# Two slot tiles of the first three batches beside the last batch's routing, and the first batches' routing inside attention's last pairs

## The reference

```python
# q, k, v: [4 batches, 8 heads, 576, 64]
scores = scale * q @ k.T                                  # per head
scores = where(scores >= max(scores) - tau, scores, -1e9)
attn = softmax(scores) @ v
x = attn.transpose(0, 2, 1, 3).reshape(4, 576, 512)

logits = x @ w_gate                                       # [4, 576, 8]
local_gate = sigmoid(x @ w_local)
for b in range(4):
    for s in range(576):                                  # in order of s
        fresh_e = argmax(logits[b, s])
        e = fresh_e if s == 0 or local_gate[b, s] < 0.5 else prev_e
        prev_e = e
        p = softmax(logits[b, s])
        out[b, s] = p[e] * (relu(x[b, s] @ w1[e]) @ w2[e])   # w1 [8,512,1024], w2 [8,1024,512]

theta = x @ w_theta                                       # x is out of the layer above
y = w_tok_r @ (x * cos(theta)) + w_tok_i @ (x * sin(theta))
u = x + y
return u + relu(u @ w_ch)
```

## Time and profile before

| | |
|---|---|
| median of 3 runs | 875.87 us (875.2 to 877.07) |
| profiled execution | 874.16 us |
| its span | 872.4 us, 16306 instructions |
| TensorE busy | 816.2 us (94%), mean granted clock 0.967 |
| VectorE busy | 459.9 us (53%) |
| ScalarE busy | 386.6 us (44%) |
| GpSimd busy | 506.1 us (58%) |
| attention | 0 to about 310 us |
| expert layer | about 310 to 612 us |
| mixing | about 612 to 872 us |

### The profile page before, as it was taken

One profiled execution on the slowest core, in us unless ns is written; L12 is line 12 of the kernel. 1 busy time (PEld: TensorE's weight loads), 2 busy tenths in 40 slices (PEclk: granted clock), 3 DMA queues, 4 the chain that ended last, 5 costly groups with the idle time before them and its releaser, 6 DMA issues. The chain is left out here.

```text
span 872.4 us, 16306 instructions
## 1 busy us (share of the span) xinstructions
PE 816.2 (94%) x5087; PEld 682.4 (78%) x5088; DVE 459.9 (53%) x1090; ACT 386.6 (44%) x667; POOL 506.1 (58%) x456
## 2 busy tenths in 40 slices
PE   6979999999999877999999999998589999999998
PEld 3768888878777656888888888886367999898998
DVE  5758888888879856221222122211196746645622
ACT  2657878878777642112121222111275525434310
POOL 4546766788897405464989899994285604303100
PEclk7889999999999988999999999998699999999999
DMA  6977687678865067766555545641310110110101
GB/s 178 343 179 199 161 198 202 161 193 203 218 150 141 15 218 247 241 212 216 181 187 186 188 162 186 229 141 34 115 48 8 55 56 25 51 35 1 48 9 54
DMA packets 78982, 123.71 MB, mean 142 GB/s; under 512 B 26336, under 2 KB 39904, under 8 KB 78944
## 3 DMA queue, kind: packets, MB, share of 16 engines
q1 hardware_dynamic: 69200, 100.41, 39.6%
q0 software_dynamic: 3552, 11.54, 4.6%
q10 hardware_dynamic: 6192, 11.27, 3.9%
HBM read 70.57 MB, written 24.12 MB: 109 GB/s over the span
## 5 line engine op out<-in xcount | busy, mean ns | idle before, releaser
L333 POOL TENSOR_SCALAR p_ring<-p_ring,xs_nat 128x576 f32<-128x576 f32 x144 | 105.5, 746 | 72.1 <-DVE xs_nat L439 72.1
L409 DVE TENSOR_REDUCE xs_nat<-psum 128x1 f32<-128x576 f32 x144 | 105.9, 749 | 46.6 <-PE psum L527 39.1
L527 PE MATMUL psum<-k_st,q_st 128*128 128x288 f32 x600 | 116.1, 320 | 8.6 <-issue 6.7
L1344 PE MATMUL psum<-w_split,h_hi 128*128 (+1 forms) x352 | 119.1, 410 | 5.0 <-DVE h_lo L1440 3.2
L424 DVE SCALAR_TENSOR_TENSOR p_ring<-psum,xs_nat,e_ring 128x576 f32<-128x576 f32 x144 | 114.5, 811 | 14.1 <-PE psum L573 8.9
L1322 PE MATMUL psum<-w_split,x_hi 128*128 (+1 forms) x352 | 118.2, 407 | 1.5 <-issue 1.1
L1231 POOL TENSOR_TENSOR w_split<-w_raw,w_split 128x1024 fp32r<-128x1024 f32 x48 | 115.0, 2395 | 4.0
L666 ACT ACTIVATE e_ring<-psum,xs_nat 128x576 f32<-128x576 f32 x144 | 105.5, 749 | 14.8 <-DVE xs_nat L409 14.1
L527 PEld LDWEIGHTS psum<-k_st,q_st 128*128 128x128 f32 x600 | 86.1, 193 | 20.5 <-DVE p_ring L424 10.9
L684 ACT COPY p_t<-psum 128x512 f32<-128x512 f32 x144 | 84.3, 586 | 38.6 <-PE psum L562 35.7
L1595 POOL TENSOR_TENSOR stage<-g,xs_nat 128x512 f32<-128x512 f32 (+1 forms) x20 | 27.3, 1366 | 110.2 <-ACT xs_nat L1801 110.2
(11 more groups left out here) (192 smaller groups left out, 1576.3 us busy)
## 6 DMA issues: line engine op xcount, KB each, us to landing
w_raw<-w_dram SPq DMA_DIRECT2D x48, 512.0 KB, 3.4
k_st<-k_split SPq DMA_DIRECT2D x60, 320.0 KB, 5.5
q_st<-q_split SPq DMA_DIRECT2D x60, 144.0 KB, 2.5
xs_dram<-stage SPq DMA_DIRECT2D x23, 256.0 KB, 2.5
ys_dram<-y_nat ACTq DMA_DIRECT2D x22, 256.0 KB, 2.2
xs_nat<-xs_dram ACTq DMA_DIRECT2D x21, 256.0 KB, 3.0
k_nat<-k_t_dram SPq DMA_DIRECT2D x15, 320.0 KB, 4.4
out_dram<-out_sb SPq DMA_DIRECT2D x32, 144.0 KB, 1.8
```

The lines of the kernel that those rows point to most:

```text
L333: pl.tensor_scalar(t, t, rsum[:, col:col + 1], 1.0, ALU.mult, ALU.mult).then_inc(s_norm, 1)
L409: dve.tensor_reduce(negmax[:, u % 3, 0:1], s_bank[u % 3][:, :, 0:HALF], AX.XY, ALU.max, negate=True).then_inc(s_max, 1)
L527: mm = pe.matmul(bank[:, x, 0:HALF], lhs, key[:, HALF * x:HALF * x + HALF], start=(j == 0), stop=(j == len(terms) - 1))
L1344: mm = pe.matmul(py, a[:, f, :], rhs.rearrange("p o n -> p (o n)"), start=(n == 0), stop=(n == len(terms) - 1))
```

## The change

Tile 0 and tile 1 now both come from the first three batches (`FIRST_TILES = 2`), and the first three batches' routing is done earlier:

- its four TensorE hops become groups of the ring, `("x", 0)` to `("x", 3)`: the transpose of the rows in two parts and the transpose back in pair 14, the ranks in pair 15. ScalarE copies each result into SBUF, and VectorE reads that copy. `logits` and `fresh` move from pair 14 to pair 13 on VectorE, `rows` and `follow` are in pair 14, `count` and `places` in pair 15;
- of the 15 one-hot matrices GpSimd makes 7 and VectorE 8; `first_pe` gives two tiles;
- expert 0's weight pieces are loaded two pairs later on SyncE; GpSimd splits pieces 0 to 3 in pairs 10 to 13, 4 and 5 in pair 14, and 6 and 7 behind the two fetches, and only then adds to `s_w1` and `s_w2`;
- the order at the expert layer's start is new on all engines: more products stand between the hops, `up(1)` stands before `down(0)`, `y_out(0)` before the low parts of expert 1's weights, and `weights` comes last;
- there are 27 possible slot tiles in place of 26, of which GpSimd gathers 4 to 26. On these inputs 22 are used, as before.

```diff
-SLOTS = (BATCH * SEQ + P - EXPERTS) // P + EXPERTS
+FIRST_TILES = 2
+SLOTS = (BATCH * SEQ + FIRST_TILES * P - EXPERTS) // P + EXPERTS
...
+    ROUTING = {(PAIRS - 2, "t", 0): (0, 1), (PAIRS - 2, "t", 3): (2,), (PAIRS - 1, "t", 0): (3,)}
...
-            if 9 <= p < 13:
-                load_w(p - 5)
+            if 11 <= p < 15:
+                load_w(p - 7)
...
-        for r in range(6):
-            pair(ITER - 4 + r // 2, r % 2, pieces=((1, r),))
-        pair(ITER - 1, 0, pieces=((0, 6), (1, 7)))
+        pair(ITER - 4, 0)
         routing["pool"]["constants"](pl)
+        pair(ITER - 4, 1)
+        for r in range(4):
+            pair(ITER - 3 + r // 2, r % 2, pieces=((1, r),))
+        pair(ITER - 1, 0, pieces=((2, 4), (1, 5)))
         pair(ITER - 1, 1, ahead=False)
-        pl.wait_ge(feed["raw_free"], PIECES)
...
+                if isinstance(i, int) and 2 * i + m == PAIRS - 3:
+                    routing["vector"]["logits"](dve)
                 if isinstance(i, int) and 2 * i + m == PAIRS - 2:
-                    routing["vector"]["logits"](dve)
+                    routing["vector"]["rows"](dve, 0)
                 if isinstance(i, int) and 2 * i + m == PAIRS - 1:
-                    routing["vector"]["rows"](dve, 0)
+                    routing["vector"]["count"](dve, 0)
...
+                if isinstance(i, int) and 2 * i + m == PAIRS - 3:
+                    routing["vector"]["fresh"](dve, 0)
                 if isinstance(i, int) and 2 * i + m == PAIRS - 2:
-                    routing["vector"]["fresh"](dve, 0)
+                    routing["vector"]["follow"](dve, 0)
+                if isinstance(i, int) and 2 * i + m == PAIRS - 1:
+                    routing["vector"]["places"](dve, 0)
...
+            if p == PAIRS - 2:
+                early(i, m, 0)
+                early(i, m, 1)
+            if p == PAIRS - 1:
+                early(i, m, 3)
+            if p == PAIRS:
+
+                routing["tensor"]["first"](pe)
...
-        pl.sem_inc(s_raw_free, 4 + PIECES)
-        pl.sem_inc(s_w1, 1)
-        pl.sem_inc(s_w2, 1)
+        routing["pool"]["lanes"](pl)
         for m in range(2):
             pl.wait_ge(s_xst[m], 32 + 32 * EARLY * DC // 2)
         reached(pl, "first")
-        fetch(x_first, keep["ahead"][:, 0:1], EARLY).then_inc(s_first[0], 16)
+        for j in range(FIRST_TILES):
+            fetch(direct[j], keep["ahead"][:, j:j + 1], EARLY).then_inc(s_first[j], 16)
+
+        for r in range(6, PIECES):
+            split_piece(pl, w, feed, 0, r)
+        pl.wait_ge(feed["raw_free"], 4)
+        pl.sem_inc(s_w1, 1)
+        pl.wait_ge(feed["raw_free"], PIECES)
+        pl.sem_inc(s_w2, 1)
+        pl.sem_inc(s_raw_free, 4 + PIECES)
...
-        transposes_x(0, x_first, s_first[0])
-        hop["rows"](pe, 1)
-        up(0, halves=range(1), part=range(0, 8))
-        hop["experts"](pe, 1)
-        up(0, halves=range(1), part=range(8, 12), ready=False)
-        hop["ranks"](pe, 1)
-        up(0, halves=range(1, 2), ready=False).then_inc(s_up, 1)
+        transposes_x(0, direct[0], s_first[0])
+        up(0, halves=range(1), part=range(0, 2))
+        hop["rows"](pe)
+        up(0, halves=range(1), part=range(2, 10), ready=False)
+        hop["experts"](pe)
+        up(0, halves=range(1), part=range(10, 12), ready=False)
+        up(0, halves=range(1, 2), part=range(0, 4), ready=False)
+        hop["ranks"](pe)
+        up(0, halves=range(1, 2), part=range(4, 12), ready=False).then_inc(s_up, 1)
+        transposes_x(1, direct[1], s_first[1])
         transposes_h(0)
+        up(1, halves=range(1))
+        up(1, halves=range(1, 2), part=range(0, 4), ready=False)
         hop["next"](pe)
-        down(0, part=range(0, 14))
+        up(1, halves=range(1, 2), part=range(4, 12), ready=False).then_inc(s_up, 1)
+        down(0, part=range(0, 12))
         hop["sources"](pe)
-        transposes_x(1, xs[:, 1, :], s_first[1])
-        down(0, part=range(14, 24), ready=False).then_inc(s_done, 1)
+        down(0, part=range(12, 24), ready=False).then_inc(s_done, 1)
+        transposes_x(2, direct[2], s_first[2])
+        transposes_h(1)
         reached(pe, "tables")
-        up(1).then_inc(s_up, 1)
-        transposes_x(2, xs[:, 0, :], s_first[2])
+        up(2).then_inc(s_up, 1)
+        transposes_x(3, direct[3], s_first[3])
+        down(1).then_inc(s_done, 1)
...
         r["last_logits"](v)
         r["fresh"](v, 1)
+        x_low(0)
         r["rows"](v, 1)
...
         r["sources"](v)
-        r["weights"](v)
+        y_out(0)
+        x_low(2)
         for n in range(4):
             low(n)
-        y_out(0)
-        x_low(2)
+        h_low(1)
         for n in range(4, PIECES):
             low(n)
+        x_low(3)
+        y_out(1)
+        r["weights"](v)
```

More of the change, by code:

```diff
@@ L100, in attention @@
     q_st = [sb(f"q_st{m}", [P, 2 * S + REM], F32R) for m in range(2)]
+    v_sb = [sb(f"v_sb{m}", [P, 2, KT, D], F32) for m in range(2)]
     k_st = [sb(f"k_st{m}", [P, 2, 2, REM + S], F32R) for m in range(2)]
@@ L494, in vector @@
         pair(0, 1)
-        with dve.Fori(1, ITER - 1) as i:
+        with dve.Fori(1, ITER - 2) as i:
             pair(i, 0)
             pair(i, 1)
+        pair(ITER - 2, 0)
+        pair(ITER - 2, 1)
         pair(ITER - 1, 0)
@@ L714, in pair @@
                 turned(i, m, 0)
+            if p == PAIRS - 2:
+                early(i, m, 0)
+                early(i, m, 1)
+            if p == PAIRS - 1:
+                early(i, m, 3)
+            if here:
                 exp(i, m, 6)
@@ L793, in order_consts, with route @@
     return np.concatenate([-1.0 * (k[:, None] > k[None, :]), np.tile(k + 1, (P, 1))], axis=1).astype(np.float32)
-def route(nc, d, own, place, sem, psum, lg, s_lg, x_tmp, const, order, eq, ident, keep, s_later, later_done, s_free, groups):
+def route(nc, d, own, long, late_rows, place, sem, psum, lg, s_lg, x_tmp, const, order, eq, ident, keep, s_later, later_done, s_free, groups, copied):
     _, cols = route_consts()
@@ L847, in columns, with ready @@
         return slice(ST * SPAN[last][0], ST * SPAN[last][1])
[L850 to L864, removed]
+    rows_at = (fresh_row[0:EARLY, :], psum[0:1, 6:8, :].rearrange("p a n -> p (a n)")[:, 0:SEQ])
+    experts_at = (early_experts, psum[:, 6, 0:ST])
+    ranks_at = (early_ranks[:, 0:EXPERTS * EARLY_TT], psum[:, 7, 0:EXPERTS * ST])
+    counts_at = (early_ranks[:, EXPERTS * EARLY_TT:], psum[:, 6, 32:32 + EXPERTS])
+    first_at, next_at, source_at = psum[:, 5, 0:2 * FIRST_TILES], psum[:, 7, 128:130], psum[:, 6, 64:64 + 2 * SLOTS]
+    def ready(v, last, hop, copied):
+        if last:
+            v.wait_ge(s_hop, hop)
+        else:
+            v.wait_ge(s_free, copied)
     def logits_early(v):
@@ L921, in places @@
         at = columns(last)
-        v.wait_ge(s_hop, 4 * last + 3)
-        link(v, v.tensor_tensor(sel[:, :, at], ranks_at(last), hot[last][:], ALU.mult))
+        ready(v, last, 4, copied[3])
+        link(v, v.tensor_tensor(sel[:, :, at], ranks_at[last].rearrange("p (e k) -> p e k", e=EXPERTS), hot[last][:], ALU.mult))
         link(v, v.tensor_reduce(rank[:, at], sel[:, :, at].rearrange("p e k -> p k e"), AX.X, ALU.add))
@@ L1059, in ranks_pe @@
         pe.wait_ge(s_bf, 3)
-        sums = tiles_of[last]
+        by_expert = ranks.rearrange("p (e k) -> p e k", e=EXPERTS)
         if last:
-            pe.matmul(ranks_at(1), bf["ones"][:], before[:].unsqueeze(2).to_broadcast([P, EXPERTS, n]), start=True, stop=False)
-        pe.matmul(ranks_at(last), bf["ones"][:], sums[:], start=not last, stop=False)
-        pe.matmul(ranks_at(last), bf["behind"][:], hot[last][:], start=False, stop=True)
+            pe.matmul(by_expert, bf["ones"][:], before[:].unsqueeze(2).to_broadcast([P, EXPERTS, n]), start=True, stop=False)
@@ L1065, in ranks_pe @@
+        pe.matmul(by_expert, bf["ones"][:], tiles_of[last][:], start=not last, stop=False)
+        pe.matmul(by_expert, bf["behind"][:], hot[last][:], start=False, stop=True)
         if last:
-            pe.matmul(counts_at[1], bf["ones"][:], before[:], start=True, stop=False)
-        mm = pe.matmul(counts_at[last], bf["ones"][:], sums[:, :, n - 1], start=not last, stop=True)
-        mm.then_inc(s_hop, 1)
+            pe.matmul(counts, bf["ones"][:], before[:], start=True, stop=False)
+        return pe.matmul(counts, bf["ones"][:], tiles_of[last][:, :, n - 1], start=not last, stop=True)
@@ L1074, in slots_pe @@
             n = TOKENS[k % ST]
-            if not name:
+            if not name and k in BY_POOL:
+                pe.wait_ge(s_lane, k - BY_POOL.start + 1)
+            elif not name:
                 pe.wait_ge(step, STEP[f"lane{k}"])
@@ L1405, in scalar @@
         high(0)
-        high(1)
         relu(0)
-        high(2)
+        x_high(1)
         h_high(0)
-        for r in range(3, 7):
+        for r in range(1, 5):
             high(r)
-        x_high(1)
-        high(7)
+        relu(1)
+        for r in range(5, PIECES):
```

(12 more changed lines are left out.)

265 lines of the change are left out of this document (156 added, 109 removed).

## The result

The changed kernel takes 881.34 us (median, 878.05 to 887.08), the kernel before beside it 875.12: a ratio of 1.0074, 95% interval 1.0056 to 1.0091. It is **slower**, by 6.5 us by this ratio (6.2 us between the medians), where 871.6 was forecast. The profiled execution took 881.69 us and its span is 879.8 us, 7.4 more than before.

What follows compares the result with a forecast made beforehand. TensorE was taken as full in attention and the expert loop, with room from 302 to 354 us. TensorE's 10 us gain is cut to 4.3 by gathers, stores and splits: 875.87 - 4.3 = 871.6 us, range 866.0 to 875.2.

Steps and rivals of the forecast that it cites:

- Part 1: Ring groups in attention pairs 13 to 15: attention ends 0.7 us later, bounds -1 and +7.
- The hand-overs: Four ring groups in pairs 13 to 15 wait for ScalarE's copies, 0.5 us each, 2.0 us in all.
- The credit of 1.3: In attention, about 1.3 us of waits in the last two pairs would now be covered.
- GpSimd loses pieces in pairs 8 and 9 and keeps two in pair 14; nothing: In attention, GpSimd has 2.5 us free per pair, so moving its pieces costs nothing.
- The slow rival: Attention's hand-overs cost 1.4 us each and VectorE's 3.2 us isn't covered: 2.5 us slower, 878.4 us, chance 0.10.
- the chain: Gathers, 23 stores, then loads and GpSimd's splits of expert weights; TensorE has 7.5 us slack at down(7), 4.1 at up(19).
- Part 2: Up to tile 0: up(0) starts at 312.6 us, as GpSimd's increment goes off when the last subtraction starts.
- Part 3: From up(0) to the relu of tile 2: 33.4 us, ending at 346.0, 10 us earlier.
- the 10 us: TensorE's gain at the relu of tile 2, forecast at 346.0 us where it was 355.83.
- Part 4: Expert loop: first gather 1.0 us later, TensorE waits for splits at down(7) and up(19), leaving 4.3 us gain.
- the slack of 4.1: At up(19), w1 of expert 7 is ready at 558.6 us, and TensorE wants it at 562.7.
- The forecast's own sign of being wrong: If attention ends more than 2 us later, the attention step is wrong.

Runs made afterwards that it cites:

- a_clear: The changed kernel with all eight pieces of expert 0's weights split in pairs 5 to 12, one each, none behind the fetches: 877.97 us, ratio 1.0028 to the kernel before.
- b_late_pieces: The kernel before with only pieces 6 and 7 split behind tile 0's fetch: ratio 1.0014 to the kernel before.
- b_shift: The kernel before with the expert layer's and the routing's tiles 32 bytes further in SBUF: ratio 0.9972 to the kernel before.
- b_shift_inter: The kernel before with tiles 32 bytes further and the loads of expert 2's w2 between the last five stores: ratio 0.993 to the kernel before.

## Why the prediction was wrong

relu(21) was forecast 4.3 us earlier and came 8.6 later, a miss of 12.9. By the steps of the prediction:

- **Part 1, attention: the step that failed.** +0.7 was forecast, +6.1 came. The hand-overs, 2.0 us, were sized nearly right: in `a_clear` the waits for the ring's copies come to 2.5. The credit of 1.3 for waits that they would cover was wrong: idle time rose by 2.4 us. Of the old waits in the last two pairs 0.49, 0.15 and 0.21 were still there, and those for VectorE and GpSimd (0.23 and 0.51) were gone, but 1.66 us of such waits stood in pair 13, to which `logits` and `fresh` had moved, where before there had been one of 0.95 for a DMA. And "GpSimd loses pieces in pairs 8 and 9 and keeps two in pair 14; nothing" counted free time per engine alone. Placed beside VectorE's moved operations the pieces cost 2.8 us, and gave back 1.4 earlier. 1.9 us were there by pair 1, and most of that is the spread between profiles. Of the miss of 5.4 us: 1.9 - 1.4 + 2.8 + (2.8 - 0.7). The slow rival (878.4, deciding from a delay of 5 us on, 0.10) came nearest and had the right route, a late end of attention that moves TensorE and the chain. But its terms didn't come: the waits of the ring were 0.2 to 0.7 us and not 1.4, and the lock wasn't in it. That it came near was in part luck.
- **Part 2, the increment: right, and not what counts.** `first_pe` took 0.94 us, the stretch to the end of the rows 4.7, tile 0 landed 3.7 us behind its fetch, all as forecast. up(0) began at 318.82, while the last subtraction ran until 317.76 + 2.35 = 320.11, so the increment goes off before the subtraction is complete, which I had counted on. The Trainium skill's page "PSUM — Partial Sum Buffer", section "Engine vs sequencer instructions", says that it goes off when the work before it is dispatched, and the trace agrees. But up(0) waited for `x_lo`, 0.9 us more: VectorE had it behind L917 and L919, the operations held up by pieces 6 and 7. I costed these pieces as a delay of the increment, and never asked what runs beside them.
- **Part 3, TensorE's gain: used up before it began.** From up(0) to relu(2) were forecast 33.4 us and came 36.5, 3.1 more. Of these 1.6 are ScalarE's: TensorE had ended up(2) at 353.30 + 0.39 = 353.69, but ScalarE began relu(2) at 355.29, and what it waited for is open. The other 1.5 I didn't take apart. With 5.4 from attention and 0.9 from `x_lo` that left 0.5 of the 10 us.
- **Part 4, the chain: the mechanism was right, its size wrong.** The waits stand at down(7) and up(19), as forecast, and the whole result is made there. Its start was forecast 1.0 us later and was 8.5: 5.4 from attention, 1.5 between `first_pe` and the last batch's rows (12.0 us; I had 10.5 from unhindered durations), 0.6 behind them. Then came what I held constant: from gather to first store 6.05 us in place of 4.07, 64.99 us of stores in place of 63.56, and in all 3.6 us more up to the split. GpSimd made up 0.7 us, where I had 1.2. So w1 of expert 7 is ready 11.4 us later, less the slack of 4.1 that is 7.3 at up(19), and the slow clock behind that wait adds 1.7, less 0.4 for shorter tiles: 8.6. The misses are 7.5 + 3.6 + 0.5 + 1.3 = 12.9, so attention's 5.4 is the largest of them and not the whole. What lengthened the way to the first store wasn't tried; the four loads of w1 of expert 2 stand just before it, and the DMA engines were busy for 0.93 of the stretch from 344.9 to 355.3 us.
- The forecast's own sign of being wrong fits: attention ended more than 2 us later, so "part 1 is".

## What to carry to other kernels

A duration read from a trace holds only beside the work that ran beside it: when VectorE's work with two SBUF inputs or GpSimd's pieces move, lay the two timelines over each other and let each small operation end with the GpSimd instruction that it meets. Where a second chain has 4 us of slack, what an edit does to the head of that chain counts first; an edit that moves only the chain (here four loads between five stores) can be worth more than the whole rearrangement of the busy engine. And a gain that vanishes should be looked for at the next wait before it is doubted: the 32 bytes gave some 4 us of TensorE's time (20 tiles at 0.22), and nothing that the times could tell until the chain was released.

## What the runs showed of the hardware

- Operations of VectorE with two inputs in SBUF, of 0.16 to 0.41 us by themselves, took up to 2.17 us beside GpSimd's instructions, and ended at most 0.3 us behind the end of the one that they met, tiny as they are. Masks with an input in PSUM took 0.81 us beside the same instructions, as before. One with a single input, the shift that makes `tile_i`, took 0.69 us in place of 0.17 beside GpSimd's scalings (`a_clear`), so a single SBUF input doesn't always keep an operation free of GpSimd.
- The products of the expert layer have a pitch that depends on where the activations' tiles begin: 12.50 us per tile (some 0.234 us per product) at offsets that divide by 64, 12.28 with 32 bytes more (0.227 for half of them). The expert layer's six tiles were moved together (and in the kernel before the routing's tiles behind them), so which of them matters is open, and no run tells the mechanism.
- The granted clock was at its half level (1.2 GHz) for the last batch's rows in six of the seven profiles of a changed kernel (1.20 to 1.25 us for five transposes, against 0.74 before), and in three of the four kernels made from the one before (`b_late_pieces`, `b_shift`, `b_shift_inter`). `b_shift` had the same wait of 1.90 us ahead of it as the kernel before, which kept the full clock; so this loss is not decided by the wait alone.
